# Pair products kept within the halves of a chunk, and scores stored in two parts

## The reference, cut to what matters

```python
def _attn_ref(r, k, v, w, u):
    for t in range(S):
        cur = np.einsum('bhd,bhe->bhde', u[None] * kt, vt)
        y[:, :, t] = np.einsum('bhd,bhde->bhe', rt, state + cur)
        state = wt[:, :, :, None] * state + np.einsum('bhd,bhe->bhde', kt, vt)

def _moe_ref(x, w_in, w_out):
    h = x @ w_in
    g = np.where(pos, h, np.where(neg, 0.0, (h + beta) ** 2 / (4.0 * beta)))
    return g @ w_out

def _moe2_ref(x, w_in, w_out):
    h = x @ w_in
    g = np.where(h > 0.0, h, alpha * (np.exp(np.minimum(h, 0.0)) - 1.0))
    return g @ w_out
```

## Time and profile before

| | us |
|---|---|
| median of 3 runs | 1051.62 (1051.09 to 1052.38) |
| profiled execution | 1053.15 |
| its span | 1051.4 |
| TensorE busy | 1000.0 |
| VectorE busy | 581.5 |
| ScalarE busy | 509.9 |
| GpSimd busy | 69.5 |

### The profile page before, as it was taken

One profiled execution on the slowest core, in us unless ns is written; L12 is line 12 of the kernel. 1 busy time (PEld: TensorE's weight loads), 2 busy tenths in 40 slices (PEclk: granted clock), 3 DMA queues, 4 the chain that ended last, 5 costly groups with the idle time before them and its releaser, 6 DMA issues.

```text
span 1051.4 us, 22880 instructions
## 1 busy us (share of the span) xinstructions
PE 1000.0 (95%) x10088; PEld 802.0 (76%) x10088; DVE 581.5 (55%) x794; ACT 509.9 (48%) x859; POOL 69.5 (7%) x50
## 2 busy tenths in 40 slices
PE   4467999999999999999999999999999999999998
PEld 3355788787878877787788888888888888888886
DVE  6955867776767776777654354533333333333332
ACT  1343444635463545446354676544544454544443
POOL 6962100000000000000000000000000000000000
PEclk8558999999999999999999999999999999999999
DMA  8315023012203020311024000000000000000000
GB/s 309 108 54 211 2 98 116 32 56 83 77 32 137 1 87 23 137 54 54 6 88 177 35 31 31 1 31 31 31 31 1 31 31 30 27 5 1 31 1 30
DMA packets 24689, 61.65 MB, mean 59 GB/s; under 512 B 2448, under 2 KB 6928, under 8 KB 24592
## 3 DMA queue, kind: packets, MB, share of 16 engines
q1 hardware_dynamic: 24592, 60.20, 15.8%
HBM read 50.76 MB, written 9.44 MB: 57 GB/s over the span
## 4 chain that ended last, share of the span: by engine, by line
PE 91%; POOL 4%; DMA 2%; SPq 1%; ACT 1%; DVE 1%; issue 0%; ACTq 0%; DVEq 0%; POOLq 0%
PE down_banks L440 39%; PE up_bank L440 29%; PE g_banks L440 16%; PE y_bank L440 5%; POOL win_lo L380 2%; POOL wout_lo L380 2%; PE y_bank L495 1%; DMA scratch<-w_in_dram 1%; DMA att<-kT_dram 1%; SPq L283 1%; PE y_bank L561 1%; POOL ynat L405 0%; POOL r_nat L396 0%; DMA scratch<-w_out_dram 0%; DVE att L834 0%
## 5 line engine op out<-in xcount | busy, mean ns | idle before, releaser
L440 PE MATMUL down_banks<-g_hi,wout_lo 128*128 128x512 f32 x576 | 237.0, 411 | 0.0
L440 PE MATMUL down_banks<-g_hi,wout_hi 128*128 128x512 f32 x576 | 227.8, 396 | 0.0
L440 PE MATMUL down_banks<-g_lo,wout_hi 128*128 128x512 f32 x576 | 226.8, 394 | 0.0
L658 ACT CAST g_hi<-scratch 128x512 fp32r<-128x512 f32 x192 | 119.3, 622 | 213.9 <-PE down_banks L440 128.2
L899 DVE TENSOR_TENSOR g_lo<-scratch,g_hi 128x512 fp32r<-128x512 f32 x192 | 132.9, 692 | 109.5 <-ACT g_hi L658 107.3
L440 PE MATMUL up_bank<-x_hi,win_lo 128*128 128x512 f32 x432 | 174.1, 403 | 2.0 <-DVE x_lo L905 2.0
L440 PE MATMUL up_bank<-x_lo,win_hi 128*128 128x512 f32 x432 | 171.3, 397 | 0.0
L440 PE MATMUL up_bank<-x_hi,win_hi 128*128 128x512 f32 x432 | 171.1, 396 | 0.0
L440 PEld LDWEIGHTS down_banks<-g_hi,wout_lo 128*128 128x128 f32 x576 | 108.2, 188 | 26.3
L440 PEld LDWEIGHTS down_banks<-g_hi,wout_hi 128*128 128x128 f32 x576 | 108.1, 188 | 26.3
L440 PEld LDWEIGHTS down_banks<-g_lo,wout_hi 128*128 128x128 f32 x576 | 108.4, 188 | 21.7
(11 more groups left out here) (82 smaller groups left out, 1083.7 us busy)
## 6 DMA issues: line engine op xcount, KB each, us to landing
att<-rT_dram SPq DMA_DIRECT2D x12, 512.0 KB, 3.6
att<-kT_dram SPq DMA_DIRECT2D x12, 512.0 KB, 5.1
att<-wT_dram SPq DMA_DIRECT2D x12, 512.0 KB, 6.4
r_nat<-rN_dram SPq DMA_DIRECT2D x12, 384.0 KB, 6.8
k_nat<-kN_dram SPq DMA_DIRECT2D x12, 384.0 KB, 8.1
att<-vN_dram SPq DMA_DIRECT2D x12, 384.0 KB, 7.3
x_dram<-r_nat SPq DMA_DIRECT2D x18, 256.0 KB, 2.3
ynat<-x_dram SPq DMA_DIRECT2D x6, 768.0 KB, 4.4
```

The source lines that it names most:

```text
L440: return nc.tensor.matmul(out, lhsT, rhs, start=start, stop=stop, **kw)
L658: return nc.scalar.copy(out, in_)
```

## The change

At levels 0 to 4 each half of the keys meets only the steps r of its own half: the moving side has 32 columns in place of 64. The products of two head pairs (the parities of j) are interleaved in PSUM, so a level fills 512 elements a partition in place of 1024. The score tile has two parts: within the halves (elements 0 to 1023: keys of a half against steps of the same half) and across (1024 to 2047: all keys against the steps of the second half). Level 6 writes across for the first half of the keys; ScalarE copies within to across for the second half of the keys, 64 partitions by 1024 elements. In `attend` the first half of the steps contracts only the 64 keys of the first half, the second half all 128. Only the first part is cleared by POOL, TensorE does not wait for it, and VectorE waits for the state's clearing at its first use.

```diff
-NMASKED = [1] * (NL - 2) + [2, 2]
+NMASKED = [1] * (NL - 2) + [2, 3]
...
+        def odd_steps(g, l, a, j, h):
+
+            steps = slice(j * CH, (j + 1) * CH) if l == NL - 1 else slice(j * CH + h * HALF, j * CH + (h + 1) * HALF)
+            return both_levels(r_[g][a * PAD:(a + 1) * PAD, steps], 2 ** l)[:, :, 1, :]
+
+        def within_halves(g):
+
+            return a_[g][:, 0:NA // 2]
+
+        def across_halves(g):
+
+            return a_[g][:, NA // 2:NA]
+
+        def head_columns(ap, a, j):
+
+            return ap.rearrange("p (a j t parity) -> p a j t parity", a=2, parity=2, t=HALF)[:, a, j // 2, :, j % 2]
...
             for g in range(2):
-                nc.gpsimd.memset(a_[g], 0.0)
+                nc.gpsimd.memset(within_halves(g), 0.0).then_inc(zeroed, 1)
...
                         for h in range(2):
-                            out = product_banks(k, g)[h * HALF:(h + 1) * HALF, a, j * PAD:(j + 1) * PAD]
-                            last = mm(out.rearrange("p (n m s) -> p s n m", m=2 ** l, s=2),
-                                      keys[:, h * HALF:(h + 1) * HALF], odd_steps(g, l, a, j))
+                            s0, s1 = h * HALF, h * HALF + (HALF if l < NL - 2 else HALF // 2)
+                            out = product_banks(k, g)[s0:s1, a, j // 2 * PAD:(j // 2 + 1) * PAD]
+                            last = mm(out.rearrange("p (t parity) -> p t parity", parity=2)[:, :, j % 2],
+                                      keys[:, s0:s1], odd_steps(g, l, a, j, h))
...
                     for a in range(2):
-                        n, e = a * GP + j, slice(j * E2 + a * D, j * E2 + (a + 1) * D)
-                        for h in range(2):
-                            hs = slice(h * HALF, (h + 1) * HALF)
-                            last = mm(y[hs, i * E2 + a * D:i * E2 + (a + 1) * D], steps_of_half(g, n, h), v_[g][:, e],
-                                      start=k == 0 and i == a == 0, stop=i == HP - 1 and a == 1,
-                                      skip_group_check=True)
...
+                        last = mm(y[0:HALF, es], head_columns(within_halves(g)[0:HALF, :], a, j), v_[g][0:HALF, e],
+                                  start=first, stop=final, skip_group_check=True)
+                        if final:
+                            last.then_inc(y_filled, 1)
+                        last = mm(y[HALF:P, es], head_columns(across_halves(g), a, j), v_[g][:, e],
+                                  start=first, stop=final, skip_group_check=True)
+                        if final:
+                            last.then_inc(y_filled, 1)
...
-            pe.wait_ge(zeroed, 1)
...
+                if l == NL - 1:
+                    act.wait_ge(masked[g], masked_after(k, NL - 2))
+                    copy(across_halves(g)[HALF:P, :], within_halves(g)[HALF:P, :]).then_inc(masked[g], 1)
+                    act.wait_ge(g_filled[g], k * NFILL + 4 * l + 4)
+                    later = across_halves(g)[0:HALF, :].rearrange("p (a x parity) -> p a x parity", a=2, parity=2)
+                    for parity in range(2):
+                        copy(later[:, :, :, parity], products[parity * HALF:(parity + 1) * HALF, :, :]).then_inc(masked[g], 1)
+                    return
...
                 elif l < NL - 2:
                     m = 2 * 2 ** l
                     nc.vector.copy_predicated(
-                        a_[g].rearrange("p (n two m) -> p n two m", two=2, m=m)[:, :, 1, :],
-                        masks[:, l:l + 1, :].broadcast_to([P, 2 * GP, HALF]),
-                        products.rearrange("p (n m) -> p n m", m=m)).then_inc(masked[g], 1)
+                        within.rearrange("p a j (n two m) -> p a j n two m", two=2, m=m)[:, :, :, :, 1, :],
+                        masks[:, l:l + 1, :].broadcast_to([P, GP, HALF]),
+                        products.rearrange("p a j (n m) -> p a j n m", m=m)).then_inc(masked[g], 1)
...
+                if k == 0:
+                    dve.wait_ge(zeroed, 3)
...
-            dve.wait_ge(zeroed, 1)
+            dve.wait_ge(zeroed, 2)
```

More of the change, by code:

```diff
@@ L463, in pair_products @@
                             out = product_banks(k, g)[half, a, j // 2 * PAD:(j // 2 + 1) * PAD]
-                            last = mm(out, keys[:, 0:HALF], odd_steps(g, l, a, j))
+                            last = mm(out, keys[:, 0:HALF], odd_steps(g, l, a, j, None)[:, 0, :])
                             if j >= GP - 2:
@@ L518, in attend @@
                     for a in range(2):
-                        n, e = a * GP + j, slice(j * E2 + a * D, j * E2 + (a + 1) * D)
-                        for h in range(2):
-                            hs = slice(h * HALF, (h + 1) * HALF)
-                            last = mm(y[hs, i * E2 + a * D:i * E2 + (a + 1) * D], steps_of_half(g, n, h), v_[g][:, e],
-                                      start=k == 0 and i == a == 0, stop=i == HP - 1 and a == 1,
-                                      skip_group_check=True)
-                            if i == HP - 1 and a == 1:
-                                last.then_inc(y_filled, 1)
+                        e = slice(j * E2 + a * D, j * E2 + (a + 1) * D)
+                        es = slice(i * E2 + a * D, i * E2 + (a + 1) * D)
+                        first, final = k == 0 and i == a == 0, i == HP - 1 and a == 1
+                        last = mm(y[0:HALF, es], head_columns(within_halves(g)[0:HALF, :], a, j), v_[g][0:HALF, e],
[6 more added lines that the diff above has]
+                            last.then_inc(y_filled, 1)
             def state_step(k, b):
@@ L808, in level @@
             def level(k, g, l):
-                products = product_banks(k, g).rearrange("p a x -> p (a x)")
+                products = product_banks(k, g)[:, :, 0:GP // 2 * PAD].rearrange("p a (j x) -> p a j x", j=GP // 2)
+                within = within_halves(g).rearrange("p (a j x) -> p a j x", a=2, j=GP // 2)
                 dve.wait_ge(g_filled[g], k * NFILL + 4 * l + 4)
@@ L814, in level @@
                     nc.vector.tensor_tensor(
-                        a_[g].rearrange("p (n t two s) -> p n t two s", n=2 * GP, two=2, s=2)[:, :, :, 1, :],
-                        products.rearrange("p (n t s) -> p n t s", n=2 * GP, s=2),
-                        masks[:, 0:1, :].bitcast(F32).rearrange("p l (t s) -> p l t s", s=2)
-                        .broadcast_to([P, 2 * GP, CH // 4, 2]), ALU.mult).then_inc(masked[g], 1)
+                        within.rearrange("p a j (t two s) -> p a j t two s", two=2, s=2)[:, :, :, :, 1, :],
+                        products.rearrange("p a j (t s) -> p a j t s", s=2),
+                        masks[:, None, 0:1, :].bitcast(F32).rearrange("p a j (t s) -> p a j t s", s=2)
+                        .broadcast_to([P, 2, GP // 2, HALF // 2, 2]), ALU.mult).then_inc(masked[g], 1)
                 elif l < NL - 2:
@@ L998, in level_masks @@
     column = np.arange(CH)
[L999 removed]
+    s, t = np.arange(P)[:, None] % HALF, (column // 2)[None, :]
     parts = []
```

30 lines of the change are left out of this document (5 added, 25 removed).

## The result

| | before | after |
|---|---|---|
| median of 4 runs, us | 1051.36 (1049.66 to 1052.38) | 1142.96 (1126.97 to 1150.38) |
| ratio | | 1.077 (1.068 to 1.085) |
| span of the profiled execution, us | 1051.4 | 1124.8 |
| TensorE busy, us | 1000.0 | 1080.6 |
| VectorE busy, us | 581.5 | 552.5 |

The change makes the kernel slower by 7.7%. This ratio leaves out the two slowest of the four runs, 1149.10 and 1150.38 us, which are over 1.5% above the fastest; with them in, the medians are 8.7% apart. The forecast was 1126 us.

What follows compares the result with a forecast made beforehand. TensorE, never resting in the loop, was taken as the bound. The profiled span of 1051.4 us plus 0 for levels, 65 for loop outputs and 10 for startup gave 1126.4 us, range 1072 to 1150.

Steps and rivals of the forecast that it cites:

- Rival A: Attention outputs on TensorE: every change of tiling is paid, 1126 us, from 1089 to 1162; chance 0.66.
- rival D: Loop outputs: many short stays lower the granted clock, 40 to 100 us on top, 1166 us or more; chance 0.07.
- The outputs: Attention output in the loop: alternating 64x64 and 128x64 tilings add 0.81 us per head pair, 65 us in all.
- The split that the prediction made: Each stay in a tiling in the outputs: 0.14 us fixed plus two unpaired rounds, 0.12 us, so 0.26 us.
- Rival B: Outputs: only tiles sharing columns wait for each other, two changes per head pair paid, about 1077 us; chance 0.18.
- The levels: 50 levels in the loop on TensorE: halved moving columns gain 0 us, with 21 us as the far end.
- The reading of the state step: State step, 64 weight columns and 48 moving: a round of 0.059 us, so fewer moving columns buy nothing.
- Rival C: Levels and outputs: tilings run together free, rounds shrink with moving columns, 1028 us at full price; chance 0.06 of faster.
- The startup: Before the loop: longer outputs add 13 us, smaller memsets and score writes return 3, so +10 us, between +2 and +14.
- ScalarE and VectorE: In the loop: ScalarE's new copies, about 1.05 us each, and VectorE's score writes, 0.69 us, both change the time by 0.
- the cover that the prediction named: ScalarE's new copy mostly passes while TensorE is still in that level's slot; without this cover it costs 10.5 us.

Runs made afterwards that it cites:

- half_weights: Changed kernel with 32 instead of 64 key columns as weights at levels 1 to 4, half of those products left out: 1129.04 us, one run.
- rows64_alone: Kernel before with one edit, the output matmul of the first half of the steps contracting only 64 keys: 1139.26 us, ratio 1.084.
- by_pair: Changed kernel with each head pair's two 64x64 output tiles ahead of both 128x64 tiles, 8 tiling changes an output: 1097.90 us, ratio 1.045.

## Why the prediction was right, step by step

**The forecast.** 1126 us against a profiled execution of 1126.97 us, and a median of 1142.96 inside the range of 1072 to 1150; one run, 1150.38, lies just above it. Rival A, every change of tiling is paid, is what happened. That the profiled execution came within 1 us is luck: outputs 3.4 us under the forecast, levels 1.5 under and layer 2 2.2 under stand against startup 1.5 over, the copy's wait 1.2 and one stretch at the lower clock. The median's distance from the forecast, 17 us, would be six or seven more such stretches; no trace of a run near the median was kept, so that is an estimate from the 2.5 us of each. It is A with a part of rival D.

**The outputs.** Forecast 4.88 us from 1.2 us per head pair, measured 4.83; forecast +65 us in the loop, measured +61.6. The split that the prediction made, 0.12 us of unpaired rounds and 0.14 us fixed, is borne out by reordering: 0.13 us per change, and 0.95 us that stays with one change. It was read from three rows that show no such pattern, so its fit was not certain beforehand.

**Rival B.** It forecast 2.9 us per output. Tiles that share no columns paid as much as the others. The rule of the Trainium skill that the prediction weighed (TensorEngine Tiling (Array Packing), Key Properties: a change of the tiling mode drains TensorE) agrees with these runs, in which every change is paid. The price of one here is 0.13 to 0.14 us.

**The levels.** Forecast 0, with 21 us as the far end; measured -1.5 us. The reading of the state step was right, and half_weights shows its reason: the weights' width sets the round. Rival C falls with it.

**The startup.** Forecast +10 us, measured +11.5, but with other terms. Outputs 2 and 3 were put at +5.5 and +3.2 us, one stretched by the lower clock and one not. Both took about 5.7 us, +4.0 and +4.7. The state steps behind them take 1.09 us, near the 1.02 and 0.99 us of the earlier trace rows at the lower level and far from the 0.61 in the loop, so both ran at that pace. The recorded clock is 1.00 there, but rows64_alone has 0.50 with the same lengths. Scaling the whole stay by 1.74 was the error: a stay took 5.66 / 16 = 0.35 us there and 0.25 in the loop, 1.4 times. by_pair's last startup output has 8 stays of four records in place of 16 of two:

```profile
79.23 4.47 PE L446 MATMUL y_bank<-att 64*64 64x48 f32 x29
83.37 0.34 PE L446 MATMUL g_banks<-att,k_nat 128*64 128x48 f32 x1
```

It takes 4.14 us, so a change costs (5.66 - 4.14) / 8 = 0.19 us there, 1.5 times its price in the loop. And the last output did not get back to full speed, as it had before. What the cleared tiles and VectorE gave back was not separated.

**ScalarE and VectorE.** Forecast 1.05 and 0.69 us, measured 1.05 and 0.73. Forecast cost of the copy 0, measured 1.4 us once. It is the level behind level 6 in one chunk, which waits for level 6's copies, and these stand behind the new one; the cover that the prediction named was there in all other places. VectorE's 29 us were worth nothing to the loop, as said.

**The clock.** "Granted clock 1.00 throughout the loop, else D": this failed in part. The prediction let D happen at every output or not at all, 40 to 100 us with a chance of 0.07. It happened at some outputs and not at others, and differently in each run, and cost from some 2 us in the profiled execution to 23 us more in the longest. The step that failed is that a rival was priced at its full extent only; a part of it added to A was the likelier case and, at some 12 us, would have put the forecast near 1138.

## What to carry to other kernels

A shorter contraction is not less work for TensorE when it makes the matmul another tiling than its neighbours: eight matmuls of 64 rows in place of 128 in an output saved no round and cost 3.08 us, 2.1 for 16 changes of tiling and, as worked out, 0.96 for tiles left without a partner. Before cutting rows or columns of small matmuls, look in the timeline which of the two operands sets the round (two rows of different widths and equal length tell it), keep one tiling for each run of matmuls, and count the tiles that run side by side. An engine that is busy 100% in both profiles can still do a tenth less: compare the instruction counts of equal windows.

## What the runs showed of the hardware

- A change between the tilings 64x64 and 128x64 costs 0.13 to 0.14 us in these fp32 streams, whether or not the tiles share columns; 0, 1, 8 and 16 changes gave outputs of 1.75, 2.84, 3.81 and 4.83 us.
- With weights of 64 columns a level took 1.10 us with 64 moving columns and 1.07 with 32; with weights of 32 columns 0.69.
- TensorE counted as busy without a gap can still be granted half its clock: stretches of 6.8 us at 1.2 GHz that begin in or behind outputs of 4.83 us with 16 changes, none with 8 changes and 3.81 us. Each cost about 2.5 us. The cause of the fall in one run and not in the next stays open.
- At the lower pace of the startup a change cost 0.19 us, against 0.13 in the loop.
- The mean granted clock of a span doesn't by itself tell its time: the kernel before took 1048.6 to 1053.5 us at 0.966 to 0.997.
- A predicated copy of 512 elements took 723 ns on 64 partitions and 731 ns on 128: two half-height writes cost nearly twice one of full height.
